# Shorter key tiles, weight loads in other places of the queue, slot folds by transposes and a vector sum, and an output in tiles of 128 rows

## Time and profile before

| | before |
|---|---|
| median of three runs | 348.76 us |
| profiled execution, own time | 347.07 us |
| span in the profile, first to last instruction | 345.3 us |
| attention | about 0 to 117 us |
| router | 117 to 142 us |
| experts | 142 to 183 us |
| feed-forward | 185 to 338 us |
| last store and end | 338 to 345.3 us |

### The profile page before, as it was taken

How to read it: one execution, slowest core, us unless ns; L and a number is a source line. 1 busy time by engine, 2 the same in 40 slices (tenths; PEclk the granted TensorE clock), 3 DMA queues, 4 the chain that set the end, 5 groups by cost and what they waited for, 6 DMA issues and landing times.

```text
span 345.3 us, 7949 instructions
## 1 busy us (share of the span) xinstructions
PE 321.7 (93%) x2985; PEld 227.1 (66%) x2985; DVE 207.0 (60%) x426; ACT 138.7 (40%) x292; POOL 77.9 (23%) x88
## 2 busy tenths in 40 slices
PE   7789999999999898979898999999999999999991
PEld 4467767777777683433423468888888888888880
DVE  3758978988986455320511885566666556566660
ACT  1445765756667331010302655452224332532520
POOL 0516556465455000000000886300000000000000
PEclk9989999999999999899999999999999999999997
DMA  7998998999999996679999800030003000300202
GB/s 256 365 345 293 364 301 343 361 302 370 341 383 424 419 391 250 249 309 370 421 376 387 328 0 2 0 122 3 0 0 122 2 0 0 124 1 0 93 4 65
DMA packets 22420, 73.23 MB, mean 212 GB/s; under 512 B 7220, under 2 KB 8180, under 8 KB 18676
## 3 DMA queue, kind: packets, MB, share of 16 engines
q1 hardware_dynamic: 21348, 72.31, 56.3%
q0 software_dynamic: 896, 0.23, 0.3%
q10 hardware_dynamic: 144, 0.26, 0.2%
HBM read 68.08 MB, written 4.46 MB: 210 GB/s over the span
## 4 chain that ended last, share of the span: by engine, by line
PE 77%; DVE 8%; DMA 5%; issue 3%; SPq 2%; ACT 1%; DVEq 0%
PE ps L801 17%; PE ps L798 17%; PE ps L716 5%; PE ps L540 5%; PE ps L585 4%; PE ps L775 4%; PE ps L745 4%; DMA qT<-q_t 3%; PE ps L577 3%; DMA vg<-vg_t 3%; PE ps L556 2%; PE ps L635 2%; PE ps L550 2%; PE ps L531 2%; DVE sc L1058 2%
## 5 line engine op out<-in xcount | busy, mean ns | idle before, releaser
L801 PE MATMUL ps<-wlo,gg 128*128 128x512 f32 x204 | 80.5, 395 | 0.0
L798 PE MATMUL ps<-whi,gg 128*128 128x512 f32 x204 | 80.2, 393 | 0.0
L1209 DVE SCALAR_TENSOR_TENSOR nt<-uu,ps 128x512 f32<-128x512 f32 (+2 forms) x80 | 48.5, 607 | 49.5 <-ACT uu L960 48.4
L960 ACT ACTIVATE uu<-ps 128x512 f32<-128x512 f32 (+2 forms) x80 | 42.8, 537 | 84.7 <-PE ps L775 81.2
L438 POOL TENSOR_TENSOR sc<-sc,mx 128x640 f32<-128x640 f32 x32 | 40.1, 1254 | 54.6 <-DVE mx L1063 54.6
L1220 DVE TENSOR_TENSOR gg<-nt,ps 128x512 fp32r<-128x512 f32 (+2 forms) x80 | 47.9, 600 | 0.1
L798 PEld LDWEIGHTS ps<-whi,gg 128*128 128x128 f32 x204 | 38.4, 188 | 8.8
L801 PEld LDWEIGHTS ps<-wlo,gg 128*128 128x128 f32 x204 | 38.3, 188 | 8.0
L1058 DVE TENSOR_TENSOR sc<-ps,cst 128x640 f32<-128x640 f32 x32 | 26.2, 819 | 8.1 <-PE ps L540 4.2
L775 PE MATMUL ps<-cT,Pst 128*128 128x512 f32 (+2 forms) x80 | 29.0, 366 | 0.6 <-DVE gg L1220 0.5
L585 PEld LDWEIGHTS ps<-vv,eT 128*64 128x64 f32 x512 | 18.7, 138 | 15.8 <-issue 13.1
(11 more groups left out here) (122 smaller groups left out, 425.1 us busy)
## 6 DMA issues: line engine op xcount, KB each, us to landing
ring<-moe_w SPq DMA_DIRECT2D x6, 2048.0 KB, 9.1
kT<-k_t SPq DMA_DIRECT2D x16, 640.0 KB, 6.9
w<-moe_w SPq DMA_DIRECT2D x5, 2048.0 KB, 10.6
w<-moe_w SPq DMA_DIRECT2D x10, 1024.0 KB, 9.0
vv<-v_t SPq DMA_DIRECT2D x8, 1170.0 KB, 8.4
qT<-q_t SPq DMA_DIRECT2D x16, 256.0 KB, 6.1
win<-moe_w_in SPq DMA_DIRECT2D x4, 1024.0 KB, 17.0
wout<-moe_w_out SPq DMA_DIRECT2D x4, 1024.0 KB, 14.9
```

The lines of the kernel that those rows point to most:

```text
L798: pe.matmul(o, g, hi, start=(c == 0), stop=False)
L801: mm = pe.matmul(o, g, lo, start=False, stop=(c == NC - 1))
L960: nc.scalar.activation(uu[c % 2][:, 0:width], cols(h_bank(i, c), width), ACT.Square, scale=(1.0 / 3) ** 0.5).then_inc(square_ready, 1)
L1209: nc.vector.scalar_tensor_tensor(out=nt[c % 2][:, 0:width], in0=uu[c % 2][:, 0:width], scalar=1.0, in1=cols(h_bank(i, c), width), op0=ALU. ...
```

## The change

- `kT` is 832 columns: nine pieces of 64 keys with the 32 global keys between neighbours, so that span t is columns 96t to 96t + 160. Mask and exponentials follow the new column order. `qT` has four buffers, and the waits ahead of the query loads are five score counts lower. In the first batch queries 2 are loaded ahead of keys 3.
- `vg` is stored with the head inside the block, so a row of a `vg` load is 260 neighbouring elements and no longer four runs of 65.
- `w2` of experts 0 to 2 is loaded in the attention loop, between queries 3 and values 1.
- `fold` is four transposes; the sum over the four groups and the copy are one VectorE reduction. The second fold uses bank 3.
- `turn_c` 2 and 3 take the place of `stay_awake` in the second layer, `turn_c` 4 stands behind it. VectorE copies `hidT` right after `both_halves(0)`.
- `w2[6]`, `w2[7]` and `w_in` have other homes, and with them other places in the order of loads: half 0 of `w2[7]` now comes ninth after `hidden_half_used`, where it came seventh.
- The output is a sequence of 17 tiles of 128 rows. SyncE stores both of the last tiles. The host puts the rows in order.

```diff
@@ -32,13 +32,12 @@
-a = np.concatenate([np.arange(128), np.full(32, -1)])[None, :]
+a = np.concatenate([np.arange(64), np.full(32, -1), np.arange(64, 128)])[None, :]
 seen = (a < 0) | ((q <= a) & (a <= q + 2 * WINDOW))
...
 for j, m in enumerate((first, seen, seen, last)):
-    m = np.roll(m, 32, axis=1) if j % 2 else m
     c[:, C_MASK + 160 * j:C_MASK + 160 * (j + 1)] = np.where(m, 0.0, MASKED / scale)
@@ -102,8 +101,8 @@
-kT = [place(f"kT{n}", [P, 8, 160], F32) for n in range(4)]
-qT = [place(f"qT{n}", [P, SL], F32) for n in range(2)]
+kT = [place(f"kT{n}", [P, 832], F32) for n in range(4)]
+qT = [place(f"qT{n}", [P, SL], F32) for n in range(4)]
 qgT = place("qgT", [P, 4, SG], F32)
@@ -158,13 +157,13 @@
 w1_home = slabC[0:3] + slabB[0:1] + [X0] + slabB[2:4] + slabC[0:1]
-w2_home = slabC[3:6] + slabB[1:2] + slabC[1:5]
+w2_home = slabC[3:6] + slabB[1:2] + slabC[1:3] + slabB[0:1] + slabC[3:4]
 w1s = [nc.alloc_sbuf_tensor_at(f"w1_{e}", [P, 4, FE], F32, offset=w1_home[e]) for e in range(NE)]
...
 assert slabB[1] - slabB[0] == 4 * SLAB
-win = place("win", [P, 4, FF], F32, slabB[0])
+win = [place(f"win{n}", [P, 4, 512], F32, (slabB[1], slabC[0])[n // 2] + 8192 * (n % 2)) for n in range(4)]
 wout = place("wout", [P, NC, DM], F32, slabB[2])
@@ -274,11 +273,10 @@
-out_b = out.rearrange("(b s) d -> b s d", b=NB)
+out_tiles = out.rearrange("(n p) d -> n p d", p=P)
...
 def out_tile(i, t):
-    b, r = (i - 1, t) if not isinstance(i, int) else divmod(FIRST[i - 1] + t, 4)
-    return out_b[b, SG + P * r:SG + P * (r + 1), :]
+    return out_tiles[4 * (i - 1) + t if not isinstance(i, int) else FIRST[i - 1] + t]
@@ -298,12 +296,12 @@
 sp.wait_ge(scores_ready, U * (i - 1) + GQ[pr // 2] + 1)
-sp.dma_start(kT[pr][:].rearrange("p t n -> p (t n)"), k_t[i - 1, pr]).then_inc(qk_loaded[pr], 16)
+sp.dma_start(kT[pr][:], k_t[i - 1, pr]).then_inc(qk_loaded[pr], 16)
...
-sp.wait_ge(scores_ready, U * (i - 1) + (7, 9, 12, 14)[pr])
-sp.dma_start(qT[pr % 2][:], q_t[i - 1, pr]).then_inc(qk_loaded[pr], 16)
+sp.wait_ge(scores_ready, U * (i - 1) + (2, 4, 7, 9)[pr])
+sp.dma_start(qT[pr][:], q_t[i - 1, pr]).then_inc(qk_loaded[pr], 16)
@@ -314,7 +312,7 @@
 for j in range(4):
-    sp.dma_start(vg[qd][SG * j:SG * j + SG, :, j, :], vg_t[i - 1, qd]).then_inc(v_loaded[qd], 16)
+    sp.dma_start(vg[qd][SG * j:SG * j + SG, j, :, :], vg_t[i - 1, qd]).then_inc(v_loaded[qd], 16)
@@ -325,8 +323,8 @@
 keys(1, 2)
+queries(1, 2)
 keys(1, 3)
-queries(1, 2)
 queries(1, 3)
@@ -342,9 +340,8 @@
     queries(i + 1, 3)
+    load_w2(sp, i - 1, w2_loaded, ring2[:, bass.ds(i - 1, 1)])
     values(i + 1, 1)
-for e in range(3):
-    load_w2(sp, e, w2_loaded, ring2[:, e:e + 1])
@@ -377,17 +374,23 @@
 half_w1(1)
+half_w2(6, 0)
 half_w2(4, 1)
+half_w2(5, 1)
+half_w2(6, 1)
 sp.wait_ge(slot_out_ready, 1)
-half_w2(6, 0)
 half_w2(7, 0)
-for e in (5, 6, 7):
-    half_w2(e, 1)
-
-for n in range(4):
+half_w2(7, 1)
+
+def load_win(n):
     f = slice(512 * n, 512 * n + 512)
-    sp.dma_start(win[:, :, f], w_in.rearrange("(p c) f -> p c f", c=4)[:, :, f]).then_inc(win_loaded[n], 16)
+    sp.dma_start(win[n][:], w_in.rearrange("(p c) f -> p c f", c=4)[:, :, f]).then_inc(win_loaded[n], 16)
+
+load_win(0)
+load_win(1)
 sp.wait_ge(hidden_ready, 2)
+load_win(2)
+load_win(3)
 for n in range(4):
@@ -406,8 +409,9 @@
+store(5, 0)
 sp.wait_ge(last_copied, 1)
-sp.dma_start(out_b[:, 0:SG, :], oo[1][:]).then_inc(out_stored[1], 16)
+sp.dma_start(out_tile(5, 1), oo[1][:]).then_inc(out_stored[1], 16)
 for t in range(4):
@@ -515,8 +519,7 @@
-a = 160 * t - SG * (t // 2 % 2)
-return kT[pr][:].rearrange("r t n -> r (t n)")[:, a:a + 160]
+return kT[pr][:, 96 * t:96 * t + 160]
@@ -526,7 +529,8 @@
 r = slice(64 * (j % 2), 64 * (j % 2) + 64)
-keys = kT[pr][r, 7, 64:64 + SG] if part else kT[pr][r, 0:8:2, 0:P]
+own = kT[pr][r, 0:768].rearrange("r (b n) -> r b n", n=96)[:, :, 0:64]
+keys = kT[pr][r, 768:768 + SG] if part else own
 o = ps[32 * j:32 * j + 32, bank + part, 0:SG if part else 512]
@@ -537,7 +541,7 @@
 o = ps[64 * (t % 2):64 * (t % 2) + 64, 2 * par + j // 2, 160 * (j % 2):160 * (j % 2) + 160]
-mm = pe.matmul(o, qT[pr % 2][r, 64 * t:64 * t + 64], seen_keys(pr, t)[r], start=True, stop=True)
+mm = pe.matmul(o, qT[pr][r, 64 * t:64 * t + 64], seen_keys(pr, t)[r], start=True, stop=True)
 if t == 7:
@@ -574,7 +578,7 @@
 pe.wait_ge(gprobsT_copied, U * i + k + 1)
-pe.matmul(cols(6 + k % 2, 4 * (D + 1)), et[:, 512:640], vg[qd][:, h].rearrange("p j d -> p (j d)"),
+pe.matmul(cols(6 + k % 2, 4 * (D + 1)), et[:, 512:640], vg[qd][:, :, h, :],
           start=True, stop=False, skip_group_check=True)
@@ -688,8 +692,7 @@
 for c in range(4):
-    mm = pe.matmul(cols(dst_bank, 32, 32 * c), v[:, c, :], cst[:, C_FOLD:C_FOLD + 32],
-                   start=True, stop=True)
+    mm = pe.transpose(cols(dst_bank, P, P * c), v[:, c, :], ident)
 mm.then_inc(s, 1)
@@ -729,8 +732,6 @@
 mm.then_inc(hiddenT_ready, 1)
-for q in range(2, NG if g else 2):
-    turn_c(q)
 pe.wait_ge(hiddenT_copied_act, g + 1)
@@ -739,15 +740,17 @@
         if g and c == 4:
-            stay_awake(2, 4, cst)
+            turn_c(2)
+            turn_c(3)
             pe.wait_ge(w2_half_loaded[1], 64)
...
     mm.then_inc(slot_out_ready, 1)
+turn_c(4)
 pe.wait_ge(so_copied, 1)
-fold(so, 7, soT_ready)
+fold(so, 3, soT_ready)
@@ -821,7 +824,7 @@
 for c in range(4):
-    mm = pe.matmul(ps[32 * c:32 * c + 32, n, :], soT[:, c, :], win[:, c, 512 * n:512 * n + 512],
+    mm = pe.matmul(ps[32 * c:32 * c + 32, n, :], soT[:, c, :], win[n][:, c, :],
                    start=True, stop=True)
@@ -869,10 +872,10 @@
 low = sc[head_of(k)[1]]
-local = bass.AP(tensor=low[:].tensor, offset=low[:].offset, ap=[low[:].ap[0], [320, 2], [192, 2], [1, P]])
-both = low[:].rearrange("p (b n) -> p b n", b=2)[:, :, P:P + 2 * SG]
-nc.scalar.activation(e[:, 0:512].rearrange("p (b a n) -> p b a n", b=2, a=2), local, ACT.Exp, scale=SCALE)
-nc.scalar.activation(e[:, 512:640].rearrange("p (b n) -> p b n", b=2), both, ACT.Exp, scale=SCALE
+local = bass.AP(tensor=low[:].tensor, offset=low[:].offset, ap=[low[:].ap[0], [160, 4], [96, 2], [1, 64]])
+shared = low[:].rearrange("p (j n) -> p j n", j=4)[:, :, 64:96]
+nc.scalar.activation(e[:, 0:512].rearrange("p (j a n) -> p j a n", j=4, a=2), local, ACT.Exp, scale=SCALE)
+nc.scalar.activation(e[:, 512:640].rearrange("p (j n) -> p j n", j=4), shared, ACT.Exp, scale=SCALE
                      ).then_inc(exp_ready, 1)
@@ -909,8 +912,6 @@
 nc.scalar.activation(cc[:], cc[:], ACT.Exp).then_inc(c_exp_ready, 1)
-act.wait_ge(slotsT_ready, 1)
-nc.scalar.copy(slotT[:].rearrange("p c s -> p (c s)"), cols(7, P)).then_inc(slotsT_copied, 1)
 def high_c(q):
@@ -930,10 +931,8 @@
     nc.scalar.copy(hidT[:, 4:8, :].rearrange("p c f -> p (c f)"), cols(3, 512)).then_inc(hiddenT_copied_act, 1)
-    for q in range(2, NG if g else 2):
-        high_c(q)
-act.wait_ge(soT_ready, 1)
-nc.scalar.copy(soT[:].rearrange("p c s -> p (c s)"), cols(7, P)).then_inc(soT_copied, 1)
+for q in range(2, NG):
+    high_c(q)
 act.wait_ge(hidden_ready, 2)
@@ -1020,8 +1019,6 @@
 results(5, 0)
-act.wait_ge(out_copied, tiles_before(5) + 1)
-act.dma_start(out_tile(5, 0), oo[0][:]).then_inc(out_stored[0], 16)
@@ -1139,6 +1136,9 @@
 nc.vector.tensor_scalar(slots[:], cols(4, 512), rD[:, 1:2], None, ALU.mult).then_inc(slots_ready, 1)
+dve.wait_ge(slotsT_ready, 1)
+nc.vector.tensor_reduce(slotT[:], cols(7, 512).rearrange("p (c g s) -> p c s g", g=4, s=32),
+                        AX.X, ALU.add).then_inc(slotsT_copied, 1)
 dve.wait_ge(c_exp_ready, 1)
@@ -1164,8 +1164,6 @@
                                op0=ALU.mult, op1=ALU.add).then_inc(cT_ready, 1)
-if q + 2 < NG:
-    spread_c(q + 2)
@@ -1176,18 +1174,25 @@
         both_halves(0)
-        both_halves(1)
     dve.wait_ge(hiddenT_ready, g + 1)
...
     nc.vector.tensor_copy(hidT[:, 0:4, :].rearrange("p c f -> p (c f)"), cols(2, 512)).then_inc(hiddenT_copied_dve, 1)
-    for q in range(2, NG if g else 2):
-        both_halves(q)
     if g == 0:
...
         spread_c(1)
+both_halves(1)
+spread_c(2)
+spread_c(3)
+both_halves(2)
+spread_c(4)
+both_halves(3)
 dve.wait_ge(slot_out_ready, 2)
 nc.vector.tensor_copy(so[:], cols(5, 512)).then_inc(so_copied, 1)
+dve.wait_ge(soT_ready, 1)
+nc.vector.tensor_reduce(soT[:], cols(3, 512).rearrange("p (c g s) -> p c s g", g=4, s=32),
+                        AX.X, ALU.add).then_inc(soT_copied, 1)
+both_halves(4)
 dve.sem_inc(negtanh_ready, NC)
@@ -1306,8 +1311,8 @@
 padded = np.concatenate([kg, k, np.zeros_like(kg)], axis=3)
-spans = [padded[..., 64 * t:64 * t + P] for t in range(8)]
-k_t = np.concatenate([np.concatenate([s, kg], axis=3) for s in spans], axis=3)
+pieces = [padded[..., 64 * t:64 * t + 64] for t in range(9)]
+k_t = np.concatenate([a for piece in pieces for a in (piece, kg)][:-1], axis=3)
@@ -1343,4 +1348,6 @@
 program(nc, *args)
-return launch(nc, [arrays], core_ids=[0]).results[0]["out"]
+rows = launch(nc, [arrays], core_ids=[0]).results[0]["out"]
```

(3 more changed lines are left out.)

## The result

The changed kernel took 339.12 us (median of four runs, 337.41 to 340.17) against 348.69 us: a ratio of 0.9728, interval 0.9683 to 0.9773, or 9.5 us less. The forecast was 336 us with a range of 333 to 340.5. The direction and the range held; of 12.9 us summed, 9.5 came. A second set of runs of the same kernel (e11) gave 339.52 us, ratio 0.9769 (0.9721 to 0.9817). A ratio leaves out the runs that lie more than 1.5% above the fastest of their kernel, so it isn't always the quotient of two medians.

A forecast was written before the change was run, and what follows sets the result against it. TensorE, busy 93% of the span, was taken as the bound, with DMA just keeping up. Gains of 5.73 + 0.92 + 0.55 + 0.9 + 0.98 + 3.8 = 12.9 us took 348.76 to 335.9, 336 us; range 333 to 340.5.

The forecast's parts named there:

- Attention: Attention start: 0.75 + 2.30 + 1.59 + 1.09 = 5.73 us gained, bounds 3 and 6; loop loads charged 0.
- C: Start of attention: wait at 18.67 only changes its releaser, clock falls as before; 339.8 us, chance 0.1.
- E: Attention loop: DMA queue doesn't keep up, 4.8 us lost, 341 us; chance 0.07 of part, 0.03 of loss beyond 12.9.
- 0.75 us from less data ahead of the constants: Start of attention: 229 KB less queued ahead of the constants moves VectorE's first mask 0.75 us earlier, bounds 0 and 1.0.
- terms of 2.30 and 1.59 us: Start of attention: TensorE's wait for queries 2 goes (2.30 us), and the half clock after it at 20 to 22 us (1.59).
- Folds: First and second fold: four transposes plus a VectorE reduction gain 0.92 us and 0.98 us.
- Group 1: Second layer's start: TensorE ready at 170.7, waits 1.4 us for half 0 of w2[7]; gain 0.55, bounds -0.5 and 2.05.
- Rival B: Group 1: a new half-clock stretch follows the wait for w2[7], price 1.6 us; 337.5 us, chance 0.15.
- `stay_awake` in the middle: Middle of group 1's second layer: stay_awake's 1.92 us replaced by eight transposes of 1.02 net; gain 0.9 us.
- End: Last store lands 2.2 us after issue instead of 6.0, sixteen engines instead of four; gain 3.8 us, low bound 3.0.
- Rival D: End: last store stays slow because the two stores meet or shape isn't the cause; 339.7 us, chance 0.05.
- Rival A: Group 0: the second half-clock stretch, costing 1.7 us, goes too; 334.2 us, chance 0.15.

The follow-up runs named there:

- e11: The changed kernel unaltered, run a second time: 339.52 us, ratio 0.9769 to the kernel before.
- e2: Kernel before with only the attention part (832-column key tiles, four query tiles, new vg layout, w2 of experts 0 to 2 in the loop): ratio 0.9883, 343.3 us.
- e4: Kernel before with only turn_c 2 and 3 for stay_awake, turn_c 4 behind the second layer, hidT copied early; old load order: ratio 0.9955.
- e5: Changed kernel with half 0 of w2[7] issued seventh after hidden_half_used again: ratio 0.961, 335.28 us.
- e6: e5 with a stay_awake of two TensorE instructions in each of three gaps around hid and hidT: ratio 0.9592, 333.34 us.
- e1: Kernel before with only the output in 17 tiles of 128 rows and both last stores on SyncE: ratio 0.9888, 343.36 us.
- e3: Kernel before with only the two folds as four transposes and a VectorE reduction: ratio 0.9963.
- e10: e6 with one more stay_awake between the second fold's transposes and TensorE's wait for VectorE's sum: ratio 0.9638, 334.87 us.

## Why the prediction came out as it did

- **Attention, right in mechanism, 0.8 us too much in the profile.** Both waits and the half-clock stretch at 20 us went, and the loop's queue kept up at the worked-out rate; rivals C and E didn't come about. The step that failed is the first, 0.75 us from less data ahead of the constants. It measured 0.11 us, at the first mask (8.10 to 7.99) and at scores 2 (10.96 to 10.85). The constants came earlier by 0.15 us in the median of all profiles, less than their spread. And where they are early, TensorE is late next: in the changed kernel the mask waits for the scores of unit 0, which end at 7.76, because TensorE's own first four matmuls hold it until 5.92 (3.78 us for the four, 1.98 later at full clock). In six of the nine profiles with the short tile the mask waits for TensorE, in three for the constants. The prediction named "what is late next" for the second wait and not for the first. Why 229 KB less in the queue bring so little is open. The terms of 2.30 and 1.59 us were read from one execution; by the medians of e2's paragraph all of attention is worth 4.3 us, 1.4 less than summed.
- **Folds, right.** 0.88 us each in the profile, 0.92 and 0.98 summed.
- **Group 1, the step that failed.** Its price of the wait for `w2[7]` was that of the standstill, 1.4 us (1.9 measured, and more in other executions), with the 32 matmuls behind it at full clock. Rival B, at 0.15, said that a half-clock stretch would follow; it did in five profiles out of five, and 1.70 us (5.34 - 3.64) are its price in the changed kernel, near the 1.6 that the rival named. The evidence was there before: the one other DMA wait of that length in the trace, 2.30 us, was followed by such a stretch. The prediction gave it a chance and left it out of the sum. The Trainium skill, "TensorE: Matmul & The Clock Gate", section "HAM oscillation — how this bites in real kernels", describes the same sequence, bursts of matmuls that start at the low clock behind a DMA wait, for waits of about 3 to 5 us. The traces agree on the sequence, and here idle times from 2.22 us on were enough (see the last section).
- **`stay_awake` in the middle, right.** 1.92 us gone, 1.02 to 1.03 us of transposes in its place.
- **The load order, right as a loss.** The prediction said that the early start of the second layer would be mostly lost to the new order. e4 and e5 show 2 us for the start with half 0 of `w2[7]` in its old place. What it didn't see is that the old order has a loss of its own: in e4 1.85 us come back as a wait in the middle of the layer, in e5, which moves this one load alone, 0.68 us.
- **End, right in six profiles of nine.** The store in four blocks ran at a DMA share of 0.25, the one of 128 rows at up to 0.95 (e6, 329 to 330 us); 3.9 us by timing (e1, 1.8 to 6.0). The profiled execution of the changed kernel showed 1.85 only, and a reading of that one profile would have called this step wrong. Rival D, a last store that stays slow, came in part in three profiles.
- **Rival A** (group 0's stretch gone) didn't come about in the profile. Others of the same kernel (e11) and of the kernel before with one part (e1, e2, e3) have none there, so it comes and goes with the execution.

Summed with what this pair of profiles showed, and with 3.8 us for the end, 12.9 - 0.8 (start) - 0.3 (folds, start of the layer) - 1.7 (clock behind the wait) is 10.1 us, against 9.5 measured with an interval of 7.9 to 11.1. The time fell into the upper part of the forecast range, which the prediction had drawn for rivals B, C and D.

## What to carry to other kernels

Price a wait like these, which stop TensorE for 2.2 us or more, with the slow matmuls behind it, here another 1.4 to 2.5 us; a load that moves two places back in a queue can bring such a wait. When a layer starts earlier, look at every later load of that layer too: e4's start came 2 us earlier and its middle waited 1.85. When an edit frees a start, ask what else ends within a microsecond of it. One profile is one execution: terms of 1 to 3 us (a store's completion, a clock stretch, the length of a wait) want several profiles or the timed runs before they are summed or called right or wrong.

## What the runs showed of the hardware that was not expected

- All seven times that TensorE stood idle for 2.2 us or more behind a DMA (2.30 in the kernel before and 2.22 in e4 near 18 us, 2.40 to 3.67 in the five above) a half-clock stretch followed or had begun. Of the two DMA waits between 1.5 and 2 us (1.63 in e1, 1.85 in e4) neither was followed by one within 3 us.
- Half-clock stretches came in most profiles (e6 and e10 have none before the last store), at different places from one kernel to the next. The kernel before varied from 344.24 to 353.57 us over 23 runs on one chip. With short matmuls in the gaps of group 0 and 1 (e6) three of four runs had a mean clock of 1.000.
- A store of 256 KB from 128 rows that had nothing behind it completed 2.2 to 4.3 us after its issue; the same amount in four blocks of 32 rows took 6.0 us in the kernel before, with a DMA share of 0.25. In the changed kernel the data was through 1.6 us after the issue (share 0.02 from 334 us on) and the completion came 2.7 us later; in e5 the data was through 1.9 us after the issue and the completion came 0.6 us later.
